# First feed-forward block in tiles of 512 tokens instead of 384, in products of 256 columns

## What is computed

```python
h = x @ w_in
g = np.maximum(h, 0.0) + alpha * np.minimum(h, 0.0)
x = g @ w_out
h = x @ w2_in
g = np.where(h > 0.0, h, np.exp(np.minimum(h, 0.0)) - 1.0)
out = g @ w2_out
```

## Time and profile before

| | us |
|---|---|
| median of three runs (lowest, highest) | 895.4 (894.45, 896.81) |
| the profiled execution, its own time | 895.38 |
| its span, first to last instruction | 893.3 |

### The profile page before, as it was taken

One profiled execution on the slowest core, in us unless ns is written; L12 is line 12 of the kernel. 1 busy time (PEld: TensorE's weight loads), 2 busy tenths in 40 slices (PEclk: granted clock), 3 DMA queues, 4 the chain that ended last, 5 costly groups with the idle time before them and its releaser, 6 DMA issues.

```text
span 893.3 us, 18782 instructions
## 1 busy us (share of the span) xinstructions
PE 885.6 (99%) x7401; PEld 861.8 (96%) x7401; DVE 536.3 (60%) x1033; ACT 301.1 (34%) x693; POOL 288.8 (32%) x444
## 2 busy tenths in 40 slices
PE   8999999999999999999999999999999999999998
PEld 7899999999999999999999999999999999999998
DVE  6676667555665354464465476666865657766563
ACT  5633344223422232232232133223442324423233
POOL 5999972222221045364376531100011100000000
PEclk9999999999999999999999999999999999999999
DMA  9894522222210026346262243443454444643411
GB/s 173 201 207 132 149 56 60 53 56 56 70 26 14 22 87 185 118 129 186 86 236 72 60 153 118 119 118 119 130 182 123 116 125 119 189 118 119 121 45 72
DMA packets 117814, 100.91 MB, mean 113 GB/s; under 512 B 63952, under 2 KB 80352, under 8 KB 117728
## 3 DMA queue, kind: packets, MB, share of 16 engines
q1 hardware_dynamic: 116512, 99.41, 39.4%
q10 hardware_dynamic: 1216, 0.30, 0.2%
HBM read 80.29 MB, written 19.40 MB: 112 GB/s over the span
## 4 chain that ended last, share of the span: by engine, by line
PE 84%; DVE 0%; ACT 0%; issue 0%
PE ps L271 19%; PE ps L272 19%; PE ps L273 19%; PE ps L281 7%; PE ps L283 7%; PE ps L285 7%; PE ps L556 1%; PE ps L596 1%; PE ps L532 1%; PE ps L543 1%; PE ps L584 1%; PE ps L564 1%; PE ps L572 1%; PE ps L552 0%; ACT xT L1091 0%; DVE common L365 0%
## 5 line engine op out<-in xcount | busy, mean ns | idle before, releaser
L273 PE MATMUL ps<-common,w_hi 128*128 128x384 f32 x768 | 258.2, 336 | 0.0
L272 PE MATMUL ps<-common,w_hi 128*128 128x384 f32 x768 | 258.1, 336 | 0.0
L272 PEld LDWEIGHTS ps<-common,w_hi 128*128 128x128 f32 x768 | 144.6, 188 | 0.0
L273 PEld LDWEIGHTS ps<-common,w_hi 128*128 128x128 f32 x768 | 144.3, 188 | 0.0
L271 PE MATMUL ps<-common,w_out_lo 128*128 128x384 f32 x384 | 133.3, 347 | 0.2 <-DVE common L365 0.2
L271 PE MATMUL ps<-common,w_in_lo 128*128 128x384 f32 x384 | 132.6, 345 | 0.0
L361 ACT ACTIVATE common<-act_g 128x384 fp32r<-128x384 f32 x96 | 50.5, 526 | 212.9 <-PE ps L273 125.2
L1058 ACT ACTIVATE act_g<-act_g 128x384 f32<-128x384 f32 x96 | 50.4, 525 | 187.2 <-DVE act_g L1054 187.2
L281 PE MATMUL ps<-w_hi,common 128*128 128x256 f32 (+1 forms) x558 | 112.5, 280 | 0.0
L283 PE MATMUL ps<-w_out_lo,common 128*128 128x256 f32 x576 | 112.4, 276 | 0.0
L285 PE MATMUL ps<-w_hi,common 128*128 128x256 f32 x576 | 112.2, 276 | 0.0
(11 more groups left out here) (116 smaller groups left out, 1437.3 us busy)
## 6 DMA issues: line engine op xcount, KB each, us to landing
ring<-w_in_parts SPq DMA_DIRECT2D x168, 256.0 KB, 2.6
w_in_parts<-parts SPq DMA_DIRECT2D x8, 1280.0 KB, 5.7
out<-xT SPq DMA_DIRECT2D x18, 256.0 KB, 2.4
xT<-in_moe_w_in SPq DMA_DIRECT2D x16, 256.0 KB, 4.7
xT<-in_moe_w_out SPq DMA_DIRECT2D x16, 256.0 KB, 4.7
raw<-in_moe_w_in SPq DMA_DIRECT2D x16, 256.0 KB, 6.3
w_in_parts<-parts SPq DMA_DIRECT2D x8, 512.0 KB, 3.1
w_stage<-in_moe_w_out SPq DMA_DIRECT2D x16, 256.0 KB, 2.7
```

What stands on the lines that cost most here:

```text
L272: pe.matmul(psum, l_hi, r_lo, start=False, stop=False)
L273: return pe.matmul(psum, l_hi, r_hi, start=False, stop=stop)
```

## The change

The first ffn is tiled by 512 tokens: four tiles of 512 and one of 256 (`width(T)`), five in all. In the wide tiles every product goes through `three_in_halves`; in the last through `three`, whose matmuls are then 256 columns wide. `XW` becomes 32. The low part of x is written over x itself (`x_lows` has the place of `xT`), so PE reads it in blocks of 32 tokens. The two g buffers and one of the two activation buffers move (`g_parts`, `act_odd`), with one more wait in the last tile (`moved`). The mixed tiles are still three, with one batch's attention in each. The rest tiles are one of 512 and one of 256 in place of three of 384, so the steps of w2_in get new places (`RAW_BEHIND`, `SUM_BEHIND`), and so do the x operands of the second ffn (`FIRST_SPLITS`). The chunks of w2_out are loaded and split in the order in which the rounds use them (0, 8, 1, 9, ...); SP loads eight of them ahead of `ring` slot 12 where it loaded fourteen.

```diff
-    XW = 96
+    XW = 32
...
+    WIDE = 512
+    TILES = -(-B * S // WIDE)
     TOK = 384
-    TILES = B * S // TOK
...
+    def width(T):
+        return min(WIDE, B * S - WIDE * T)
...
+        with ExitStack() as place_of_x:
+            x_lows = keep("x_lows", [P, B * NXB, KC, XW], F32R, place_of_x)
         xT = keep("xT", [P, B * NXB, KC, XW])
...
-                pe.matmul(psum[:, cols], l_hi, r_lo[:, cols], start=False, stop=False)
+                pe.matmul(as_in(r_lo, psum[:, cols]), l_hi, some(r_lo, cols), start=False, stop=False)
...
+        def three_of(T):
+
+            return three_in_halves if width(T) == WIDE else three
...
-            last = three(pe, bank_h(h_banks, c), (w_hi[:, 0, c, cols], w_in_lo[:, c, cols]),
-                         (buf.x_hi[:, kk, :, :].rearrange("p g q -> p (g q)"),
-                          buf.x_lo[:, kk, :, :].rearrange("p g q -> p (g q)")), kk == 0, kk == KC - 1)
+            last = three_of(T)(pe, bank_h(h_banks, T, c), (w_hi[:, 0, c, cols], w_in_lo[:, c, cols]),
+                               (buf.x_hi[:, kk, 0:width(T)], x_lo_tile(T, kk)), kk == 0, kk == KC - 1)
...
-            last = three(pe, ps[:, m, 0:TOK], (w_hi[:, 1, c, cols], w_out_lo[:, c, cols]),
-                         (buf.g_hi[:, b, :], buf.g_lo[:, b, :]), c == 0, c == FC - 1)
+            last = three_of(T)(pe, ps[:, m, 0:width(T)], (w_hi[:, 1, c, cols], w_out_lo[:, c, cols]),
+                               (g_hi(T, c), g_lo(T, c)), c == 0, c == FC - 1)
...
-            dve.tensor_tensor(buf.x_lo[:, kk, :, :], x_tile(T, kk), buf.x_hi[:, kk, :, :].bitcast(F32),
-                              ALU.subtract).then_inc(x_split, 1)
+            dve.tensor_tensor(x_lo_tile(T, kk), x_tile(T, kk),
+                              in_blocks(buf.x_hi[:, kk, 0:width(T)].bitcast(F32)), ALU.subtract).then_inc(x_split, 1)
...
+            if moved(T, c):
+                dve.wait_ge(g2_done, T * FC)
...
+            W2_ORDER, W2_SOON = [HC * half + j for j in range(HC) for half in range(2)], 8
...
-            FIRST_SPLITS = {3: [0, 5], 6: [1, 6], 9: [2], 12: [3], FC - 1: [4]}
+            FIRST_SPLITS = {3: [0], 6: [1], 10: [5], 11: [2], 13: [6, 3], FC - 1: [4]}
...
-                    pe.wait_ge(w2_split, chunk + 1)
+                    pe.wait_ge(w2_split, W2_ORDER.index(chunk) + 1)
...
-                for c in range(2, FC - 2):
-                    load_w2_out(c)
+                for n in range(2, W2_SOON):
+                    load_w2_out(n)
                 for s in range(RING, NPR * LAST_J):
                     load_parts(s)
-                    if s in (RING + 1, RING + 4):
-                        load_w2_out(FC - 2 + (s - RING) // 4)
+                    if (s - RING) % 3 == 0 and W2_SOON + (s - RING) // 3 < FC:
+                        load_w2_out(W2_SOON + (s - RING) // 3)
...
-                            batch = ((t + 2) * TOK - 1) // S
+                            batch = ((t + 2) * WIDE - 1) // S
...
+                RAW_BEHIND = [*((MIXED, c) for c in (2, 4, 6, 9, 11, 13)), (MIXED + 1, 1), (MIXED + 1, 5)]
+                SUM_BEHIND = [*((MIXED, c) for c in (3, 5, 8, 10, 12, 14)), (MIXED + 1, 3), (MIXED + 1, 7)]
...
-                            if t < TILES - 1 and at % 4 == 1:
-                                raw_hi((t - MIXED) * KC + at // 4)
-                            elif t < TILES - 1 and at % 4 == 3:
-                                sum_hi((t - MIXED) * KC + at // 4)
-                            elif t == TILES - 1:
+                            if (t, at) in RAW_BEHIND:
+                                raw_hi(RAW_BEHIND.index((t, at)))
+                            if (t, at) in SUM_BEHIND:
+                                sum_hi(SUM_BEHIND.index((t, at)))
+                            if t == TILES - 1:
...
-                for c in range(FC):
+                for n, c in enumerate(W2_ORDER):
```

120 lines of the change are left out of this document (75 added, 45 removed).

## The result

| | changed | before |
|---|---|---|
| median us (lowest, highest) | 903.03 (902.50, 903.65), four runs | 895.08 (894.45, 896.81) |
| span of the profiled execution | 900.9 | 893.3 |

The ratio is 1.0086, with a 95% interval from 1.0069 to 1.0104: slower, where faster was forecast. The granted TensorE clock is 1.00 throughout, as before, the 2.4 GHz level. The profiled execution took 903.04 us.

What follows compares the result with a forecast made beforehand. The prediction took PE to be the bound in every stretch. From 895.4 us it subtracted 7.6 (step 1), added 0.8 (step 4) and 0.1 for small boundary waits, giving 888.7 us, with a range of 887.0 to 893.3 (0.84).

Steps and rivals of the forecast that it cites:

- Step 1: First ffn: 256-column matmuls at the unit products' 113.3 ns take 391.6 us instead of 399.3, gaining 7.6 us.
- A rule against it: First ffn: the skill's N/2.4 + 2.5 ns per matmul gives 374.4 to 377.3 us, 2.9 us slower; the prediction went by the trace.
- The fixed price of a matmul belongs to the first ffn: Rival, chance 0.03: 13.3 ns is paid on each 256-column matmul too, 120.0 ns, 15.4 us slower, 911.6 us.
- Blocks are dear: Rival, chance 0.07: first ffn matmuls reading `x_lows` in blocks take longer; 13 ns each cancels the gain, 58 ns gives 922.
- The other two: Rivals: handover stops PE 2 to 5 us (0.15, 890 to 893); w2_in prepared after J=0 starts (0.03, about 894).
- Step 2: Attention, mixed tiles and alone stage: longer VectorE operations fit the room, so nothing; at worst 0.8 us in the alone stage.
- Step 3: Preparing w2_in in the shorter stretch before J=0 stays hidden: nothing, first `ring` load about 12 us ahead, ScalarE waiting 1.1 us.
- Step 4: Round J=0 shrinks to 11.4 us, less than VectorE likes; PE waits at the start of J=1, +0.8 us.
- The small waits at new boundaries, 0.1: Small waits at the three new boundaries, 0.1 us in the sum.

Runs made afterwards that it cites:

- e1_whole: The changed kernel with whole matmuls of 512 columns in the wide tiles instead of two halves of 256; 897.86 us, ratio 1.0034.
- e2_pad: The changed kernel with 64 unused bytes moving `x_his`, `common`, `g_parts` and `ring` to the remainder of `w_hi`; 915.02 us, ratio 1.0224.
- e11_halved_both: The changed kernel with each sum's first matmul also halved, `w_in_lo` 96 bytes lower, `xT` and `x_lows` 64 bytes higher; 903.11 us, ratio 1.0095.
- e12_no_blocks: As e11_halved_both, but first products' middle matmuls read `x_his` instead of `x_lows`, so nothing is read in blocks; 904.98 us (909.98, 909.63, 900.33, 899.09).
- e10_halved: The changed kernel with the first matmul of each sum cut in two as well, leaving no whole 512 there; 903.73 us, ratio 1.0099.
- m4_seed: Bare matmul streams without the computation, copying the kernels' operand orders behind one another, each group behind a pause; 256-column matmuls at 113.3 or about 118 ns.
- e5_w: The changed kernel with only `w_in_lo` moved 96 bytes lower, to remainder 0; 903.39 us, ratio 1.0092.
- e3_both: The changed kernel with `w_in_lo` 96 bytes lower and `xT` and `x_lows` 64 bytes higher, so all products have unlike remainders; 903.84 us, ratio 1.0102.
- e6_swap: The changed kernel with remainders exchanged: first ffn weights at 64, activations at 0; 902.48 us, ratio 1.0079.
- m1_streams: Bare streams of 60 matmuls, no other engine working, varying operand places, alignment and width; 256 columns took 113.3 to 120.0 ns.
- m3_grid: Bare matmul streams, remainders of the two operands varied one by one, behind pauses; 113.3 ns only when remainders differed by 64, like remainders 118.7 to 120.0.
- e9_whole_both: The changed kernel with whole matmuls of 512 in wide tiles, `w_in_lo` 96 bytes lower and `xT` 64 bytes higher; 897.4 us, ratio 1.0026.

## Why the prediction was wrong

**Step 1 failed: "226.6 ns a pair, 113.3 ns each".** I took a price from one place of the program and used it in another. Measured in the first ffn are 117.9 ns (tile 3), and the term is +8.2 us instead of -7.6. The runs show in its place that a matmul of 256 columns has two lasting prices, 113.3 and 117.8 ns, when the starts of its operands differ by 64 bytes of 128, and other prices, from 116.7 to 120.0, when they don't. The unit products are in the fast one nearly all the time, the first ffn's stream nearly never. The width pays only at the fast price: 2 x 118 = 236 ns stands against 231.1 in matmuls of 384. Slow price and fast price lie on either side of the break-even of 115.5 ns.

That the pair price is what cost the time is shown by e1_whole (5 us back with the halves alone undone) and, from the other side, by e2_pad (the unit products lose 5 ns a matmul, those of 384 3 ns, and the kernel 12 us). Two things are shown to end a fast stretch: a matmul on `x_lows`, read in blocks (5 of 5 in e11_halved_both; in e12_no_blocks, where `x_his` is read in its place, fast stretches run through the first products), and a whole matmul of 512 (e10_halved, on the unit products; 7 of 7 in the first ffn, though there `x_lows` follows at once). e12_no_blocks exchanges the place of the operand together with the blocks, so the two are not separated. `w_in_lo` at remainder 96 ended one fast stretch in the one trial of m4_seed, and moving it alone gained nothing (e5_w). The changed kernel has all three.

What begins a fast stretch is the other half. The traces of the changed kernel, e3_both to e6_swap and e10_halved to e12_no_blocks have 57 fast stretches of six matmuls or more in the first ffn, and 56 of them begin with the first product behind a burst of attention (the other one behind a whole 512). The rest tiles have no bursts, and are slow even in e12_no_blocks. Nor is it chance from one kernel to the next: the stretch at 161 us begins with the 125th product of the first ffn in the changed kernel, in e5_w and in e10_halved, and one begins with the 370th product in four of the traces. What in the restart behind a burst or a pause chooses the price stays open, and the two levels of e12_no_blocks suggest that it can differ between executions of one kernel. A first ffn that was fast throughout was never seen, so that 888.7 us could be had with it is not shown.

**A rule against it.** The Trainium skill's rule ("TensorE: Matmul & The Clock Gate", "Back-to-back issue gap") forecast slower, because a fixed part is paid more often, and slower came. Its sizes were not right: 162.5 and 109.2 ns against 173.3 and 117.9, and 898.3 us against 903.0. The section itself calls this the gap of a matmul by itself, and says that it does not fit a stream with weight loads, which the prediction left out. Nor is its reason shown. Over the columns at 2.4 GHz the measured prices leave 13.3 ns at 384, and 11.2 or 6.6 at 256, so it is no fixed part. That the direction came out is luck in so far as at the fast price it would not have. I put the rule aside since the unit products disagreed with it, and for the first ffn they were the wrong witness.

**The rivals.** "The fixed price of a matmul belongs to the first ffn" had 0.03 and 120.0 ns, 911.6 us. Its price came nearest, since 117.9 lies two thirds of the way from mine to it; I held the unit products against it, which was just the error. Its mechanism is not confirmed: the price belongs to no stage, and the unit products pay 117.7 in e12_no_blocks. "Blocks are dear" (0.07) was half right: the matmuls that read blocks take 118.8 ns, hardly more than their neighbours, where I priced them at 13 ns and more; but a fast stretch ends at them, and they cost the kernel by that. The other two did not occur.

**Step 2 held.** No wait for attention or for a split is in the list that was not there before; those for `xT` lie in the alone stage of both. The alone stage is longer by 0.6 us, within the worst case of 0.8 that I gave and took as 0. That isn't clear of noise: in the versions above, whose attention is the same, the first product starts anywhere from 35.5 to 38.6 us.

**Step 3 held.** The first load into `ring` (timeline of the queue SP, beside the earlier trace rows) and the longest wait of ScalarE for POOL's sums:

```profile
508.60 0.34 SPq L1292 DMA_DIRECT2D ring<-w_in_parts  x1
```

```profile
511.04 0.85 ACT L1031 ACTIVATE w_hi<-t_sums 128x768 fp32r<-128x768 f32 x1 [1.59 <-POOL t_sums L1697]
```

The load is 12.9 us ahead of J=0, at 521.54 (12 said); ScalarE waits 1.59 us (1.1 said), of which nothing shows in PE's waits.

**Step 4 held.** Timeline of PE in J=1, and of DVE:

```profile
533.13 0.34 PE L287 MATMUL ps<-w_hi,ring 128*128 128x384 f32 x1
...
534.64 0.40 PE L301 MATMUL ps<-w_hi,common 128*128 128x256 f32 x2
535.52 0.44 PE L287 MATMUL ps<-w_hi,ring 128*128 128x384 f32 x1 [0.48 <-DVE h_units L1102]
```

```profile
532.98 1.00 DVE L1119 SCALAR_TENSOR_TENSOR h_units<-act_g,h_units 128x384 f32<-128x384 f32 x1
533.90 1.10 DVE L1130 TENSOR_TENSOR common<-h_units,common 128x384 fp32r<-128x384 f32 x1
```

J=0 takes 533.13 - 521.54 = 11.59 us (11.4 said; the twelve second products are 0.354 us instead of 0.340). The pair at 534.64 would be over at 534.87, and the next starts at 535.52; with the late start behind it some 0.76 us are lost, where 0.8 was said. It is the product behind the first unit product of J=1, the one at 528.05 in the earlier trace rows, whose 0.98 us of margin are gone. VectorE's two operations of 1.00 and 1.10 us, beside POOL, hold it up, as the prediction had it. The small waits at new boundaries, 0.1, are not to be seen.

## What to carry to other kernels

A price read from start to start holds for the stream in which it was read: its neighbours, its operands' places, its widths. Before a whole stage is re-tiled on the strength of a few nanoseconds a matmul, run that stage's own stream once; here a gain of 2% a column hung on it, and the price moved by 4%. And read it at several places of the trace: unit products at 117.5 were there before the change. After an edit that moves buffers, look also at matmuls that the edit doesn't touch: with 64 bytes of padding they were 4% longer.

## What I had not expected of the hardware

- Matmuls of 256 columns in fp32r run at 113.3 or at 117.8 ns for long stretches, at one clock and with the same operands (m1_streams, L44 and L63). One kernel took 899 to 900 us twice and 910 us twice, which such a flip would explain (e12_no_blocks).
- In the first ffn 56 of 57 fast stretches begin directly behind a burst of attention (eight traces), and all five that reach a matmul which reads blocks end at it (e11_halved_both).
- When both operands start at the same place of 128 bytes, they take 116.8 to 120 ns and never took 113.3 (m1_streams, m3_grid, e2_pad).
- Wider ones vary less, by their length: 173.3 to 177 ns at 384 columns, 229 to 233 at 512. At 128 columns they take 111 ns (m1_streams, L59), almost as much as 256.
- Whole 512-column matmuls that read in blocks of 32 take 237 ns against 229 to 232 on plain rows (e9_whole_both), while in halves they take about 1 ns more than their neighbours.
